# A radix search whose counts take several token groups per product: radices 64 and 32 in place of 41

## The chip, the cores and the metric

One NeuronCore of a Trainium2 chip. The metric is the device time of one execution in microseconds, the median of the runs; lower is better.

## The reference

Three stages follow one another. First a linear attention with decay over 4 x 8 heads, 768 positions and 48 dimensions per head. Its output, 3072 tokens of 384 features, goes to the second stage, a mixture of 8 experts with a greedy assignment: the (token, expert) logits are taken from the largest down, and each expert takes 384 tokens at most.

```python
logits = x @ w_gate
order = np.argsort(-logits.flatten())
for idx in order:
    tok, e = (int(idx) // E, int(idx) % E)
    if assigned[tok] >= 0 or counts[e] >= cap:
        continue
    assigned[tok] = e
    counts[e] += 1
...
    h = np.maximum(x[mask] @ w1[e], 0.0)
    out[mask] = h @ w2[e]
```

The third stage is a dense layer pair with hidden size 2048, `np.maximum(x @ w_in, 0)` squared, times `w_out`.

## The kernel before

The attention runs first, in 24 units of 128 tokens (4 sequences x 6 chunks). While it runs, the third stage's weights are loaded and split into a high and a low part, so that each later product is made of three (L1194, `three`: high x high, high x low, low x high). The logits of all 3072 tokens stay in SBUF as 128 partitions x 24 units x 8 experts.

**The routing** is done in rounds, `round_steps(q)` (L720). Each round finds the next expert that fills up. Every open token has its best open expert; the round looks for the largest key (the logit's 32 bits as an ordered integer, in two halves of 16 bits) at which some expert would hold 384 tokens. The search for one 16-bit half has three steps k = 0, 1, 2 with radix T = 41 and step sizes 1681, 41 and 1. The two halves give six search steps, called 0.0 to 1.2 here. One step is this:

- `compare(half, k)` (L783) on VectorE: thresholds (`steps` at k = 0, else `steps` plus the base found so far, L795), then 0/1 for "key at least threshold" in two operations of 12 units x 41 thresholds each (L802), written to `hot`, a bf16 tile of 24 x 128 columns per partition, of which a unit uses its first 41.
- `count(q, half, k)` (L1138) on TensorE: for each of the 24 units a product of the unit's 128 columns of `hot` with its 8 columns of `openc` (which expert an open token chose), summed in PSUM (L1143), and one product of `ones` with `need8` (L1144), which brings in the tokens already held and the capacity. Row t of the result says for each expert whether it would be full at threshold t.
- `fullness` (L805) on VectorE: 1 for each threshold at which some expert is full (`gecnt`, L808, with an accumulator read).
- `add_full` (L1146) on TensorE: a product that counts these thresholds on every partition (L1149).
- `rebase` (L810) on VectorE: the new base (L814, L817).

Step 1.0 has three more operations ahead of its comparison (L788 to L792). After step 1.2 come the sum per expert, the ranks of its tokens, and a permutation of 384 token numbers, with which GpSimd gathers the rows of x.

**Order of the work.** Round 0 runs alone between the attention and the first expert, each step waiting for the one before. Then `pe.Fori(0, E - 2)` runs `expert(i, False, True)` for six experts, each together with the search for the next one; the seventh expert has a round without search, the eighth none. In `expert` (L1258) the hidden groups g = 1 to 24 come in turn, 8 of the expert's first layer and 16 of the dense one. `hidden(i, g)` (L1200) is nine products of 384 columns (3 values of d, three each); `contract(i, g)` is nine more, into the outputs. The searching parts are written between them by hand: `count` of step g - 2 stands at the end of iteration g for g = 2 to 7, `add_full` of step g - 3 inside `hidden` for g = 3 to 8, as `between`, ahead of the three products of the last d (L1206). Group 8 is the first of the dense layer, and its products of each d wait for `x2_lo_ready`. VectorE's order is in `expert` from L969 on: `low(i, g)`, the low part of hidden group g, comes ahead of the search part of the same iteration; in iteration 7 the comparison of step 1.2 comes ahead of the three low parts of the dense layer's input (L986), and the fullness test of step 1.2 behind them.

```python
for k in range(3):
    last = pool.iota(steps[:, k, :], [[STEPS[k], T]], base=0, channel_multiplier=0, **iota)
...
pool.memset(hot[:, :, :], 0.0)
```

GpSimd makes these tables at the start (L369 to L376); VectorE and TensorE wait for `made` to reach 13, which the last of the three iotas does.

Of the kernel before, what the change touches and what calls it, by code (L numbers as in the profile page):

```python
# [27 lines left out]
E = 8  # L28
# [20 lines left out]
T = 41  # L49
STEPS = [T * T, T, 1]  # L50
# [14 lines left out]
def _route_names():  # L65

    names = ["best", "is_best", "ranked", "first", "choice", "open_choice", "held", "need",
             "sign", "key", "hi_int", "hi", "lo_int", "lo"]
    for half in range(2):
        if half:  # L70
            names += ["above", "clamp", "low_key"]
        for k in range(3):
            names += [f"thr{half}{k}"] if k else []
            names += [f"ge{half}{k}a", f"ge{half}{k}b", f"full{half}{k}", f"base{half}{k}"]
# [14 lines left out]
def build(nc, tt_d, nn_d, w_d, u_d, wg_d, we_d, m2_d, out_d):  # L89
# [5 lines left out]
    with ctx:  # L95
# [17 lines left out]
        full = sb("full", [P, 1], bf16)  # L113
        ones48 = sb("ones48", [P, 2 * NU], f32)
        steps = sb("steps", [P, 3, T], f32)
# [9 lines left out]
        ge = hot[:, :, 0:T]  # L125
# [58 lines left out]
        thr = sb("thr", [P, T], f32)  # L184
        gecnt = sb("gecnt", [T, E], f32)
# [25 lines left out]
        cnt_ps, n_ps, e_ps = rt_ps[:, 0:E], rt_ps[:, 16:17], rt_ps[:, 32:32 + E]  # L211
# [128 lines left out]
        def _(pool):  # L340
# [34 lines left out]
            pool.memset(hot[:, :, :], 0.0)  # L375
# [220 lines left out]
        def _(dve):  # L596
# [123 lines left out]
            def round_steps(q):  # L720
# [62 lines left out]
                def compare(half, k):  # L783

                    key = key2 if half else key_hi
                    if half and k == 0:

                        did("above", dve.tensor_scalar(tmp[:, :], key_hi[:, :], base[0][:, 0:1], 65536.0, ALU.subtract, ALU.mult))  # L788
                        after("above")
                        did("clamp", dve.tensor_scalar(tmp2[:, :], tmp[:, :], 65536.0, -65536.0, ALU.min, ALU.max))  # L790
                        after("clamp")
                        did("low_key", dve.tensor_tensor(key2[:, :], tmp2[:, :], key_lo[:, :], ALU.add))  # L792
                        after("low_key")
                    if k:
                        did(f"thr{half}{k}", dve.tensor_scalar(thr[:, :], steps[:, k, :], base[half][:, 0:1], None, ALU.add))  # L795
                        after(f"thr{half}{k}")
                        at = thr[:, :]
                    else:
                        at = steps[:, 0, :]
                    for part, units_ in (("a", slice(0, NU // 2)), ("b", slice(NU // 2, NU))):  # L800
                        did(f"ge{half}{k}{part}",
                            dve.tensor_tensor(ge[:, units_, :], key[:, units_].unsqueeze(2).broadcast_to([P, NU // 2, T]),  # L802
                                              at.unsqueeze(1).broadcast_to([P, NU // 2, T]), ALU.is_ge))

                def fullness(half, k):  # L805

                    dve.wait_ge(counted, 6 * q + 3 * half + k + 1)
                    did(f"full{half}{k}", dve.tensor_scalar(gecnt[:, :], cnt_ps[0:T, :], 0.0, None, ALU.is_ge, ALU.max, accum_out=full[0:T, :]))  # L808

                def rebase(half, k):  # L810

                    dve.wait_ge(summed, 6 * q + 3 * half + k + 1)
                    if k:
                        did(f"base{half}{k}", dve.tensor_scalar(base[half][:, :], n_ps, float(STEPS[k]), base[half][:, 0:1],  # L814
                                                                ALU.mult, ALU.add))
                    else:
                        did(f"base{half}{k}", dve.tensor_scalar(base[half][:, :], n_ps, float(STEPS[k]), None, ALU.mult))  # L817
# [214 lines left out]
        def _(pe):  # L1032
# [105 lines left out]
            def count(q, half, k):  # L1138

                for a in range(NU):  # L1140
                    if a % (NU // 2) == 0:
                        pe.wait_ge(route_done, q * RN + DONE[f"ge{half}{k}{'ab'[a // (NU // 2)]}"])
                    pe.matmul(cnt_ps, hot[:, a, :], openc[:, a, :], start=a == 0, stop=False)  # L1143
                pe.matmul(cnt_ps, ones[:, :], need8[:, :], start=False, stop=True).then_inc(counted, 1)  # L1144

            def add_full(q, half, k):  # L1146

                pe.wait_ge(route_done, q * RN + DONE[f"full{half}{k}"])
                pe.matmul(n_ps, ones_but0[:, :], full[:, :], start=True, stop=True).then_inc(summed, 1)  # L1149
# [44 lines left out]
            def three(out, hi_w, lo_w, hi_x, lo_x, first, last):  # L1194
# [141 lines left out]
```

## Time and profile before

| what | value |
|---|---|
| median of 3 runs | 878.4 us (878.37 to 878.81) |
| the profiled execution | 878.33 us, its span 876.6 us |
| TensorE busy | 811.8 us, 93% of the span |
| VectorE busy | 551.1 us, 63% |
| ScalarE and GpSimd busy | 290.0 and 328.7 us |
| attention | about 0 to 171 us |
| round 0 and the first gather | about 171 to 213 us |
| passes over the experts | from 213 us, some 82 us each |

The span is the time from the first to the last instruction of the profiled execution. Busy time of TensorE counts overlapping products once; single products last longer than the distance from one start to the next, so costs are read from distances between starts. The row of a group of the same instructions in the timeline gives their number as x24.

### The profile page before, as it was taken

The page shows a single profiled execution, that of the slowest core. Times are in us where ns is not written, and L with a number is a line of the kernel's source. Part 1 is how long each engine was busy: PE and PEld are TensorE (multiplying, and loading weights), DVE is VectorE, ACT ScalarE, POOL GpSimd, SP SyncE. Part 2 cuts the span into 40 slices and gives each one's busy share as a digit, 9 for nine tenths or more (in the row PEclk, how much of TensorE's full clock was granted, in tenths as well). Part 3 has the DMA queues.
Part 4 walks back from the last instruction along what each step waited for, and adds up shares of the span by engine and source line. Part 5 has one row for each costly group of instructions (what it writes and reads, how often), then busy time and mean ns, then how long its engine had stood idle before and what let it go on. Part 6 is the DMA issues. An engine that isn't in the chain of part 4 may idle for free.

```text
span 876.6 us, 18438 instructions
## 1 busy us (share of the span) xinstructions
PE 811.8 (93%) x6695; PEld 777.4 (89%) x6695; DVE 551.1 (63%) x1159; ACT 290.0 (33%) x581; POOL 328.7 (37%) x312
## 2 busy tenths in 40 slices
PE   5999999624999999999999999999999999999995
PEld 4888888623899999999999999999999999999995
DVE  7999999675777458546845692678358633931210
ACT  1233332103135315422542253235314533542332
POOL 6777677203026303520541063126303520531232
PEclk9999999855999999999999999999999999999998
DMA  8776776013023001200310040022002200400000
GB/s 228 213 220 232 214 250 209 29 51 121 2 73 100 26 2 72 99 27 0 120 50 27 8 162 0 27 72 99 9 18 72 99 27 1 172 1 28 1 1 27
DMA packets 22143, 69.86 MB, mean 80 GB/s; under 512 B 3552, under 2 KB 6752, under 8 KB 22112
## 3 DMA queue, kind: packets, MB, share of 16 engines
q1 hardware_dynamic: 19040, 59.99, 21.2%
q0 software_dynamic: 3072, 9.44, 3.1%
q8 instruction: 21, 0.34, 0.2%
q14 instruction: 10, 0.08, 0.0%
HBM read 59.98 MB, written 9.44 MB: 79 GB/s over the span
## 4 chain that ended last, share of the span: by engine, by line
PE 77%; DVE 11%; issue 5%; POOL 5%; ACT 1%; DMA 0%; DVEq 0%; POOLq 0%
PE bank L1196 16%; PE bank L1197 15%; PE bank L1198 15%; PE bank L1250 8%; PE bank L1252 8%; PE bank L1251 8%; PE bank L1143 3%; DVE ks L638 2%; PE bank L1059 2%; DVE am L645 1%; DVE rs L639 1%; POOL rku L401 1%; DVE hot L802 1%; POOL kn L385 1%; POOL rk L396 1%
## 5 line engine op out<-in xcount | busy, mean ns | idle before, releaser
L469 POOL TENSOR_TENSOR h_lo<-sq,h_hi 128x384 fp32r<-128x384 f32 x128 | 152.9, 1198 | 398.2 <-DVE sq L966 398.1
L966 DVE SCALAR_TENSOR_TENSOR sq<-bank,relu 128x384 f32<-128x384 f32 x128 | 71.0, 555 | 133.6 <-ACT relu L565 133.3
L1250 PE MATMUL bank<-m_hi,h_hi 128*128 128x384 f32 x384 | 132.0, 344 | 0.0
L1196 PE MATMUL bank<-x_hi,m_hi 128*128 128x384 f32 x384 | 130.6, 340 | 0.3
L1252 PE MATMUL bank<-m_hi,h_lo 128*128 128x384 f32 x384 | 129.8, 338 | 0.0
L1251 PE MATMUL bank<-m_lo,h_hi 128*128 128x384 f32 x384 | 129.5, 337 | 0.0
L1197 PE MATMUL bank<-x_lo,m_hi 128*128 128x384 f32 x384 | 129.2, 336 | 0.0
L1198 PE MATMUL bank<-x_hi,m_lo 128*128 128x384 f32 x384 | 129.1, 336 | 0.0
L565 ACT ACTIVATE relu<-bank 128x384 f32<-128x384 f32 x128 | 63.0, 492 | 194.5 <-PE bank L1198 192.3
L559 ACT ACTIVATE h_hi<-bank 128x384 fp32r<-128x384 f32 x64 | 31.5, 492 | 192.1 <-PE bank L1198 192.0
L958 DVE SCALAR_TENSOR_TENSOR h_lo<-bank,h_hi 128x384 fp32r<-128x384 f32 x64 | 35.4, 554 | 72.0 <-ACT h_hi L559 72.0
L1196 PEld LDWEIGHTS bank<-x_hi,m_hi 128*128 128x128 f32 x384 | 72.3, 188 | 1.1 <-DVE x_lo L986 0.9
L264 DVE TENSOR_TENSOR w_lo<-w_raw,w_hi 128x1024 fp32r<-128x1024 f32 x47 | 72.4, 1545 | 0.4 <-ACT w_hi L541 0.4
L1251 PEld LDWEIGHTS bank<-m_lo,h_hi 128*128 128x128 f32 x384 | 72.3, 188 | 0.0
L1250 PEld LDWEIGHTS bank<-m_hi,h_hi 128*128 128x128 f32 x384 | 72.2, 188 | 0.0
L1197 PEld LDWEIGHTS bank<-x_lo,m_hi 128*128 128x128 f32 x384 | 72.2, 188 | 0.0
L1252 PEld LDWEIGHTS bank<-m_hi,h_lo 128*128 128x128 f32 x384 | 72.2, 188 | 0.0
L1198 PEld LDWEIGHTS bank<-x_hi,m_lo 128*128 128x128 f32 x384 | 72.1, 188 | 0.0
L1196 PE MATMUL bank<-x_hi,w_hi 128*128 128x384 f32 x192 | 71.1, 370 | 0.8 <-DVE x_lo L923 0.8
L567 ACT ACTIVATE h_hi<-relu 128x384 fp32r<-128x384 f32 x128 | 67.4, 527 | 4.1
L1197 PE MATMUL bank<-x_lo,w_hi 128*128 128x384 f32 x192 | 65.7, 342 | 0.0
L1198 PE MATMUL bank<-x_hi,w_lo 128*128 128x384 f32 x192 | 65.7, 342 | 0.0
(172 smaller groups left out, 1572.4 us busy)
## 6 DMA issues: line engine op xcount, KB each, us to landing
w_raw<-we_in SPq DMA_DIRECT2D x48, 512.0 KB, 4.9
nn<-nn_in SPq DMA_DIRECT2D x24, 576.0 KB, 4.1
tt<-tt_in SPq DMA_DIRECT2D x48, 192.0 KB, 4.9
m_raw<-m_in SPq DMA_DIRECT2D x12, 512.0 KB, 5.7
x_rows<-yrow SPq DMA_DIRECT2D x24, 192.0 KB, 1.9
xg<-x_rows,perm_next POOLq DMA_INDIRECT x24, 4.4
out<-xg,perm_now POOLq DMA_INDIRECT x24, 2.6
u_row<-u_in SPq DMA_DIRECT2D x1, 192.0 KB, 6.0
```

The source lines that it names most:

```text
L264: eng.tensor_tensor(w_lo[:, cols], w_raw[j % W_SLOTS][:, :], w_hi[:, cols].bitcast(f32), ALU.subtract).then_inc(w_lo_ready, 1)
L469: pool.tensor_tensor(h_lo[g % 3][:, :], sq[g % 2][:, :], h_hi[g % 3][:, :].bitcast(f32), ALU.subtract).then_inc(lo2_ready, 1)
L565: act.activation(relu[:, :], h_ps[g % 3][:, 0:CAP], ACT.Relu).then_inc(relu_ready, 1)
L567: act.activation(h_hi[g % 3][:, :], relu[:, :], ACT.Square).then_inc(h_hi_ready, 1)
L958: dve.scalar_tensor_tensor(out=h_lo[g % 3][:, :], in0=h_ps[g % 3][:, 0:CAP], scalar=0.0, in1=h_hi[g % 3][:, :].bitcast(f32), op0=ALU.max, ...
L966: dve.scalar_tensor_tensor(out=sq[g % 2][:, :], in0=h_ps[g % 3][:, 0:CAP], scalar=0.0, in1=relu[:, :], op0=ALU.max, op1=ALU.mult).then_inc ...
L1196: pe.matmul(out, hi_w, hi_x, start=first, stop=False)
L1197: pe.matmul(out, hi_w, lo_x, start=False, stop=False)
L1198: return pe.matmul(out, lo_w, hi_x, start=False, stop=last)
L1250: pe.matmul(acc_ps[t][:, 0:DM], h_hi[r][:, s], m2_hi[:, c:c + DM], start=first, stop=False)
L1251: pe.matmul(acc_ps[t][:, 0:DM], h_hi[r][:, s], m2_lo[:, c:c + DM], start=False, stop=False)
L1252: last = pe.matmul(acc_ps[t][:, 0:DM], h_lo[r][:, s], m2_hi[:, c:c + DM], start=False, stop=end)
```

## The change

The radix is no longer the same in all steps. Steps 0.0 and 1.2 have radix 64, the other four radix 32; per half 64 x 32 x 32 = 65536 thresholds. The comparison writes its results to `hot` without gaps, t columns per unit. So 128 adjacent columns hold 2 units (radix 64) or 4 (radix 32), and one product takes these with the 16 or 32 columns of `openc` of the same units. Of its result only the diagonal blocks are wanted: rows j*t to (j+1)*t with columns 8j to 8j+8. A count has 12 or 6 such products and, as before, one with `need8`, into the first 8 columns. `fullness` first copies block 0 from PSUM to `folded`, then adds the others one by one, each operation waiting for the one before, and then makes the test on `folded`. The thresholds come from one `ramp` by multiplication, at k = 0 too. `full` gets a second column, for radix 64. The memset of `hot` goes. In `three` the call of `between` stands behind the first of the three products of the last d, one product later than before.

```diff
-T = 41
-STEPS = [T * T, T, 1]
+T = [[64, 32, 32], [32, 32, 64]]
+STEPS = [[1024, 32, 1], [2048, 64, 1]]
...
-            for k in range(3):
-                last = pool.iota(steps[:, k, :], [[STEPS[k], T]], base=0, channel_multiplier=0, **iota)
-            last.then_inc(made, 1)
+            pool.iota(ramp[:, :], [[1, 64]], base=0, channel_multiplier=0, **iota).then_inc(made, 1)
...
-            pool.memset(hot[:, :, :], 0.0)
...
+                    t = T[half][k]
                     if k:
-                        did(f"thr{half}{k}", dve.tensor_scalar(thr[:, :], steps[:, k, :], base[half][:, 0:1], None, ALU.add))
-                        after(f"thr{half}{k}")
-                        at = thr[:, :]
+                        did(f"thr{half}{k}", dve.tensor_scalar(thr[:, 0:t], ramp[:, 0:t], float(STEPS[half][k]), base[half][:, 0:1],
+                                                               ALU.mult, ALU.add))
                     else:
-                        at = steps[:, 0, :]
+                        did(f"thr{half}{k}", dve.tensor_scalar(thr[:, 0:t], ramp[:, 0:t], float(STEPS[half][k]), None, ALU.mult))
+                    after(f"thr{half}{k}")
+                    ge = flat[:, 0:NU * t].rearrange("p (u t) -> p u t", t=t)
...
                 def fullness(half, k):
+                    t = T[half][k]
                     dve.wait_ge(counted, 6 * q + 3 * half + k + 1)
-                    did(f"full{half}{k}", dve.tensor_scalar(gecnt[:, :], cnt_ps[0:T, :], 0.0, None, ALU.is_ge, ALU.max, accum_out=full[0:T, :]))
+                    did(f"fold{half}{k}0", dve.tensor_copy(folded[0:t, :], cnt_ps[0:t, 0:E]))
+                    for j in range(1, P // t):
+                        after(f"fold{half}{k}{j - 1}")
+                        did(f"fold{half}{k}{j}", dve.tensor_tensor(folded[0:t, :], cnt_ps[j * t:(j + 1) * t, j * E:(j + 1) * E],
+                                                                   folded[0:t, :], ALU.add))
+                    after(f"fold{half}{k}{P // t - 1}")
+                    did(f"full{half}{k}", dve.tensor_scalar(gecnt[0:t, :], folded[0:t, :], 0.0, None, ALU.is_ge, ALU.max,
+                                                            accum_out=full[0:t, t // 64:t // 64 + 1]))
...
             def count(q, half, k):
-                for a in range(NU):
+                many = P // T[half][k]
+                for a in range(0, NU, many):
                     if a % (NU // 2) == 0:
                         pe.wait_ge(route_done, q * RN + DONE[f"ge{half}{k}{'ab'[a // (NU // 2)]}"])
-                    pe.matmul(cnt_ps, hot[:, a, :], openc[:, a, :], start=a == 0, stop=False)
-                pe.matmul(cnt_ps, ones[:, :], need8[:, :], start=False, stop=True).then_inc(counted, 1)
+                    pe.matmul(cnt_ps[:, 0:many * E], flat[:, a * T[half][k]:a * T[half][k] + P],
+                              openc[:, a:a + many, :].rearrange("p u e -> p (u e)"), start=a == 0, stop=False)
+                pe.matmul(cnt_ps[:, 0:E], ones[:, :], need8[:, :], start=False, stop=True).then_inc(counted, 1)
...
                 pe.matmul(out, hi_w, hi_x, start=first, stop=False)
+                if between:
+                    between()
                 pe.matmul(out, hi_w, lo_x, start=False, stop=False)
...
-                    if between and d == DC - 1:
-                        between()
...
                     last = three(h_ps[h][:, 0:CAP], w1[:, c:c + P], w2[:, c:c + P], a1[:, d, :], a2[:, d, :],
-                                 d == 0, d == DC - 1)
+                                 d == 0, d == DC - 1, between if d == DC - 1 else None)
```

## Rows read from the trace of the kernel before

**Rows 1.** Second pass: stretch, us, PE, PEld, DVE, ACT, POOL busy, PEclk, DMA share, GB/s.
```profile
295.00:377.00 82.00, 82.00 (x624) 79.46 (x623) 52.52 (x124) 30.12 (x55) 26.39 (x23) 1.00 0.15 53
```

**Rows 2.** Timeline of TensorE, second pass, step 0.0: start us, us, engine, line, operation.
```profile
307.94 0.76 PE L1143 MATMUL bank<-openc,hot 128*128 128x8 bf16 x24
...
308.56 0.17 PE L1144 MATMUL bank<-need,ones 128*128 128x8 bf16 x1
...
309.56 0.34 PE L1198 MATMUL bank<-x_hi,w_lo 128*128 128x384 f32 x1
...
309.74 0.18 PE L1149 MATMUL bank<-full,ones_but 128*128 128x1 bf16 x1
```

**Rows 3.** Timeline of TensorE, second pass, the ranks' products.
```profile
338.54 0.20 PE L1158 MATMUL bank<-cand,before 128*128 128x48 bf16 x1
...
338.60 0.43 PE L1250 MATMUL bank<-m_hi,h_hi 128*128 128x384 f32 x1
```

**Rows 4.** Groups of VectorE by form: busy us, mean ns | idle before.
```profile
L802 DVE TENSOR_TENSOR hot<-key_hi,thr 128x492 bf16<-128x492 f32 x28 | 17.6, 673 | 0.5
...
L745 DVE TENSOR_TENSOR r<-logits,best 128x192 f32<-128x192 f32 x8 | 2.9, 358 | 0.3
```

**Rows 5.** Timeline of VectorE, second pass, steps 0.0 and 0.1.
```profile
306.27 1.25 DVE L802 TENSOR_TENSOR hot<-key_hi,steps 128x492 bf16<-128x492 f32 x2
...
308.76 0.16 DVE L808 TENSOR_SCALAR_CACHE_REDUCE gecnt<-bank 41x8 f32<-41x8 f32 x1 [0.77 <-PE bank L1144]
...
310.43 1.26 DVE L802 TENSOR_TENSOR hot<-key_hi,thr 128x492 bf16<-128x492 f32 x2
```

**Rows 6.** Timeline of TensorE and VectorE, second pass, step 1.0.
```profile
317.80 0.18 PE L1149 MATMUL bank<-full,ones_but 128*128 128x1 bf16 x1
...
318.02 0.22 DVE L814 TENSOR_SCALAR base<-bank,base 128x1 f32<-128x1 f32 x1 [1.02 <-PE bank L1149]
...
318.27 0.24 DVE L788 TENSOR_SCALAR tmp<-key_hi,base 128x24 f32<-128x24 f32 x1
...
318.98 1.26 DVE L802 TENSOR_TENSOR hot<-key,steps 128x492 bf16<-128x492 f32 x2
...
320.04 0.76 PE L1143 MATMUL bank<-openc,hot 128*128 128x8 bf16 x24
```

**Rows 7.** Timeline of VectorE ahead of the loop, small operations behind the last step.
```profile
191.07 0.17 DVE L831 SCALAR_TENSOR_TENSOR row<-bank,rank 128x8 f32<-128x8 f32 x1 [0.31 <-PE bank L1154]
...
191.27 0.16 DVE L834 TENSOR_REDUCE top<-row 128x1 f32<-128x8 f32 x1
```

**Rows 8.** Timeline of both engines, first pass, step 0.0.
```profile
224.33 1.25 DVE L802 TENSOR_TENSOR hot<-key_hi,steps 128x492 bf16<-128x492 f32 x2
...
225.63 0.37 PEld L1143 LDWEIGHTS bank<-openc,hot 128*128 128x128 bf16 x12 [0.21 <-DVE hot L802]
...
225.92 0.10 PEld L1144 LDWEIGHTS bank<-need,ones 128*128 128x128 bf16 x1
```

**Rows 9.** Timeline ahead of the loop, step 0.1: test and add_full.
```profile
177.14 0.16 DVE L808 TENSOR_SCALAR_CACHE_REDUCE gecnt<-bank 41x8 f32<-41x8 f32 x1 [0.60 <-PE bank L1144]
...
177.37 0.19 PE L1149 MATMUL bank<-full,ones_but 128*128 128x1 bf16 x1 [0.26 <-DVE gecnt L808]
```

**Rows 10.** Timeline of both engines, second pass, step 1.2.
```profile
327.98 1.26 DVE L802 TENSOR_TENSOR hot<-key,thr 128x492 bf16<-128x492 f32 x2
...
329.34 1.60 DVE L986 TENSOR_TENSOR x_lo<-bank,x_hi 128x384 fp32r<-128x384 f32 x3
...
329.67 0.76 PE L1143 MATMUL bank<-openc,hot 128*128 128x8 bf16 x24
...
331.45 0.18 PE L1149 MATMUL bank<-full,ones_but 128*128 128x1 bf16 x1
```

**Rows 11.** Timeline of the start, GpSimd and VectorE.
```profile
6.34 0.43 POOL L370 IOTA steps<- 128x41 f32 x3
...
6.89 1.61 DVE L622 TENSOR_TENSOR_SCAN powr<-w_s,powr,zeros 112x128 f32<-112x128 f32 x4 [1.35 <-POOL steps L370]
```

More of the change, by code:

```diff
@@ L72, in _route_names @@
         for k in range(3):
-            names += [f"thr{half}{k}"] if k else []
-            names += [f"ge{half}{k}a", f"ge{half}{k}b", f"full{half}{k}", f"base{half}{k}"]
+            names += [f"thr{half}{k}", f"ge{half}{k}a", f"ge{half}{k}b"]
+            names += [f"fold{half}{k}{j}" for j in range(P // T[half][k])]
+            names += [f"full{half}{k}", f"base{half}{k}"]
     names += ["at_least", "reached", "reached_sum",
@@ L112, in build @@
         ones_but0 = sb("ones_but0", [P, P], bf16)
-        full = sb("full", [P, 1], bf16)
+        full = sb("full", [P, 2], bf16)
         ones48 = sb("ones48", [P, 2 * NU], f32)
-        steps = sb("steps", [P, 3, T], f32)
+        ramp = sb("ramp", [P, 64], f32)
         rank8 = sb("rank8", [P, E], f32)
@@ L124, in build @@
         hot = sb("hot", [P, NU, P], bf16)
-        ge = hot[:, :, 0:T]
+        flat = hot[:, :, :].rearrange("p u s -> p (u s)")
         att = ExitStack()
@@ L183, in build @@
         need8 = sb("need8", [P, E], bf16)
-        thr = sb("thr", [P, T], f32)
-        gecnt = sb("gecnt", [T, E], f32)
+        thr = sb("thr", [P, 64], f32)
+        gecnt = sb("gecnt", [64, E], f32)
+        folded = sb("folded", [64, E], f32)
         base = [sb(f"base{j}", [P, 1], f32) for j in range(2)]
@@ L813, in rebase @@
                     if k:
-                        did(f"base{half}{k}", dve.tensor_scalar(base[half][:, :], n_ps, float(STEPS[k]), base[half][:, 0:1],
+                        did(f"base{half}{k}", dve.tensor_scalar(base[half][:, :], n_ps, float(STEPS[half][k]), base[half][:, 0:1],
                                                                 ALU.mult, ALU.add))
                     else:
-                        did(f"base{half}{k}", dve.tensor_scalar(base[half][:, :], n_ps, float(STEPS[k]), None, ALU.mult))
+                        did(f"base{half}{k}", dve.tensor_scalar(base[half][:, :], n_ps, float(STEPS[half][k]), None, ALU.mult))
                     after(f"base{half}{k}")
@@ L1138, in count @@
             def count(q, half, k):
-                for a in range(NU):
+                many = P // T[half][k]
+                for a in range(0, NU, many):
                     if a % (NU // 2) == 0:
                         pe.wait_ge(route_done, q * RN + DONE[f"ge{half}{k}{'ab'[a // (NU // 2)]}"])
-                    pe.matmul(cnt_ps, hot[:, a, :], openc[:, a, :], start=a == 0, stop=False)
-                pe.matmul(cnt_ps, ones[:, :], need8[:, :], start=False, stop=True).then_inc(counted, 1)
+                    pe.matmul(cnt_ps[:, 0:many * E], flat[:, a * T[half][k]:a * T[half][k] + P],
+                              openc[:, a:a + many, :].rearrange("p u e -> p (u e)"), start=a == 0, stop=False)
+                pe.matmul(cnt_ps[:, 0:E], ones[:, :], need8[:, :], start=False, stop=True).then_inc(counted, 1)
             def add_full(q, half, k):
                 pe.wait_ge(route_done, q * RN + DONE[f"full{half}{k}"])
-                pe.matmul(n_ps, ones_but0[:, :], full[:, :], start=True, stop=True).then_inc(summed, 1)
+                wide = T[half][k] // 64
+                pe.matmul(n_ps, ones_but0[:, :], full[:, wide:wide + 1], start=True, stop=True).then_inc(summed, 1)
             def expert_counts(q):
@@ L1192, in _, with three @@
                         last.then_inc(x_sum, 1)
-            def three(out, hi_w, lo_w, hi_x, lo_x, first, last):
+            def three(out, hi_w, lo_w, hi_x, lo_x, first, last, between=None):
                 pe.matmul(out, hi_w, hi_x, start=first, stop=False)
+                if between:
+                    between()
                 pe.matmul(out, hi_w, lo_x, start=False, stop=False)
```

6 lines of the change are left out of this document (3 added, 3 removed).

## The prediction

> **What bounds the kernel now.** I read the busy time by stretches first. In a full pass over one expert TensorE is busy for 82.00 of 82.00 us [rows 1], with VectorE at 52.5: there an instruction taken off TensorE is time taken off the end, as long as VectorE keeps up. Then I read the timeline of TensorE around one search step of the second pass [rows 2]. A search step is a count, VectorE's fullness test, add_full, the rebase and the next comparison; I call the six 0.0 to 1.2 (half, k). The 24 count products take 0.62 us from the first start to the start of the product with ones, 26 ns each, and add_full starts 1.18 us after the latter. Neighbouring 384-column products start 0.18 us apart. So a count costs TensorE far less than the 0.17 us that one product lasts. Last I read VectorE's side, for where it is late next: step 0.0, step 1.0, step 1.2, the first pass, and the serial search ahead of the loop.
>
> **What goes from TensorE.** Counts with radix 32 issue 6 products in place of 24, those with radix 64 issue 12. If a product of 16 or 32 columns is as dear as one of 8, a pass saves 4 x 18 + 2 x 12 = 96 products of 26 ns, 2.48 us, and six searching passes 14.9 us. Two products with 48 columns in the same stretch take 0.06 us together until the next product starts [rows 3], 30 ns each; narrower ones should lie between 26 and 30, and I take 26. At 30 the 48 that are left cost 0.2 us more a pass.
>
> **What VectorE gets.** Per comparison the elements go from 2 x 492 to 2 x 384 or 2 x 768. An operation on 192 elements lasts 358 ns and one on 492 lasts 673 [rows 4], 1.05 ns per element more; the two halves of 492 last 1.25 us together [rows 5], so the second starts 0.09 before the first one's end. That gives 0.56 us for one half with radix 32 and 1.03 for the pair, and 0.96 and 1.83 with radix 64. Steps 0.0 and 1.0 get a threshold operation that they did not have; three chained small operations ahead of step 1.0's comparison take 318.98 - 318.27 = 0.71 us [rows 6], so 0.24.
>
> The fullness test gets a fold in front: four chained operations with radix 32, two with radix 64, and the trace has none that read the counts from partitions 32, 64 or 96. From below, the nearest row is an 8-element operation that reads the PSUM bank: the one that depends on it starts 0.20 us later [rows 7]. From above, the rebase with its pointer operand gives 0.25 [rows 6]. I take 0.20, since the folds have the shape of the former and no pointer, and keep 0.25 for the range; below, nothing in the chain could be shorter than some 0.15, the 0.17 that such an operation lasts less its overlap.
>
> The Trainium skill (VectorE: DVE Perf Modes, Rules for kernel authors) speaks against a change of this sort: the count of chained VectorE operations is what matters, not their semaphores. The table in its section on the errata gives 120 cycles and the elements for a PSUM source, 133 ns here by estimate; the rows show 0.20. With its figure the search ahead of the loop would be 1.3 us shorter than below and step 1.2 some 0.13 in each pass, and the time about 872.0.
>
> **The search ahead of the loop** is serial, so each operation counts in full. After a comparison ends, the second half of the products starts 0.05 us later [rows 8] and takes 0.31, half of the 0.62 above; add_full starts 0.23 after the test [rows 9]. With radix 32: comparison -0.22, the second half of the products 12 to 3, -0.23, folds +0.80, together +0.35. With radix 64: +0.58, -0.16, +0.40, together +0.82. Four and two of them and two thresholds: 1.40 + 1.64 + 0.48 = **3.5 us lost**. The gather and the expert's load hang on its result and move with it.
>
> **The loop**, step by step.
> Steps 0.1, 0.2 and 1.1: the test starts 0.20 us after the product with ones (308.76 less 308.56) [rows 2, 5], so with the folds add_full can start 0.20 + 0.80 + 0.23 = 1.23 after it. TensorE came there after 1.18; now one 384-column product more is issued ahead of it (the call moves into three(), behind its first product), so 1.36, and the chain is hidden with 0.13 to spare. That product covers it: without it TensorE would wait 0.05. The next comparison starts 0.69 after add_full (310.43 less 309.74, and 0.06 more behind a pointer rebase) [rows 2, 5] and is done with 1.03 + 0.05 at about 1.83, ahead of the count's second half at some 2.1. So these three keep 0.46 each, 1.39.
> Step 1.0: before, the product with ones starts 2.86 us after add_full (317.80 to 320.04 and 0.62) [rows 6]; with the moved add_full and the shorter count it could be 2.86 - 0.18 - 0.46 = 2.22. But the comparison starts 1.18 after add_full, now 1.42, and 1.03 + 0.05 and three products later it is 2.58. TensorE waits 0.36 and 0.10 is left. Queued behind the comparison is the low part of hidden group 5, which is due an entire group later.
> Step 0.0: the comparison starts at 306.27 [rows 5], now at 306.51; it ends at 308.34, and the six products of the second half bring the product with ones to 308.55, against 308.56 before. The saving of 0.31 is eaten whole.
> Step 1.2: the comparison starts at 327.98 and holds VectorE until 329.72 instead of 329.24 [rows 10]. Behind it in VectorE's order are the three low parts of the second layer's input, for which TensorE waits at hidden group 8. The first now starts at 329.72 in place of 329.34, and group 8 starts about 0.3 later than it could. The three take 0.47 each and are through at 331.13, two folds bring the test to 331.53 and add_full to 331.76, against 331.45. One product less follows it, so this step **loses 0.14**. The sum over experts comes only behind the nine products of group 9 and is not held up.
> A pass so gains 0 + 1.39 + 0.10 - 0.14 = 1.35 us, six of them 8.1. In the first pass VectorE is late already: step 0.0's comparison starts at 224.33 and TensorE, waiting, reaches the product with ones at 225.92 [rows 8]. Now that is 224.33 + 0.24 + 1.83 + 0.05 + 0.16 = 226.61, another 0.69 lost. The loop gains **7.4 us**.
>
> **The start.** GpSimd makes one ramp, not three step tables: two of three iotas that take 0.43 us together go, and VectorE waits on the last of them [rows 11]. 0.28 us gained. The memset of the one-hot tile that goes lies behind that, under VectorE's own work: nothing; were it on the path it would be a gain. The pass without search and the last one have no counts.
>
> **Sum.** -0.28 + 3.5 - 7.4 = -4.2 us. The profiled execution took 878.33 us, 1.7 around its span of 876.6; it stands 0.07 under the median of the runs. I forecast **874.1 us**.
>
> **Rivals.**
> *The fold is dearer than I take it, and the kernel slower.* With a fold step of 0.20 + x, the twenty folds ahead of the loop cost 20x; in a pass the four steps with radix 32 stall by 4x - 0.13 each and step 1.2 by 2x, so six passes cost 108x - 3.1. The gain is gone at 128x - 3.1 = 4.2, x = 0.057: it decides at a step of 0.257 us. At 0.30, which reads from other partitions than it writes could cause, the time is 878.3 - 4.2 + 9.7 = 883.8. For it: no row shows such an operation, and TensorE's spare is 0.13 us. Against it: the small operations of the rows lie between 0.20 and 0.25 apart. 8 in 100.
> *No change that can be told.* A fold step of 0.25 gives 128 x 0.05 - 3.1 = +3.3, 877.4 us; products at 30 ns and waits that cost TensorE 0.1 more at each of three stalls lead there too. 13 in 100.
> *The waits that I find at steps 0.0, 1.0 and 1.2 do not cost time.* Then the whole 14.9 less 3.5 is kept with the start, 866.7 us. It would need VectorE to do 768 elements in the time of 492, for which no row speaks. 5 in 100.
> That the products are not fewer can be excluded: the loop's stride sets their number.
>
> **How the numbers follow.** My own case has 74 in 100, all of it faster by more than 0.2% (1.8 us, about what a measurement of this kernel can tell from no change). With the third rival that is 0.79 faster, 0.13 the same, 0.08 slower. The range runs from 870.7, where a fold step is 0.15 (1.0 less ahead of the loop, 0.6 less in it, from step 1.2 alone) and the waits at steps 0.0 and 1.2 halve (1.8 less), to 877.4 at a fold step of 0.25; it leaves out the first rival, the third and a sliver.
>
> **What would show it.** TensorE's counts: 12 or 6 products to a count, still 26 ns apart; in radix-32 steps 0.16 us from the first to the product with ones. VectorE: comparisons of 384 elements near 0.56 us and of 768 near 0.96; folds starting 0.20 apart. Waits of TensorE: new ones on the comparison at steps 0.0 and 1.0 of every pass (0.3 to 0.4 us), at group 8 on the low part of its input (0.3), and none at add_full in steps 0.1, 0.2 and 1.1. The search ahead of the loop from the first comparison to the last rebase longer by 3.5 us, each searching pass shorter by 1.35. A wait at add_full in every step, or folds over 0.25 apart, would make me wrong.

## The result and the profile after

The changed kernel takes 873.11 us (median of 5 runs, 873.04 to 875.22) against 878.4 (878.29 to 878.81): a ratio of 0.9948, interval 0.9936 to 0.996, so 0.5% faster. The profiled execution took 873.07 us with a span of 871.3; before it was 878.33 with 876.6. The runs of the changed kernel and of some variants fall on two levels some 2 us apart, so small differences are read from the profiled executions, which but for six_idle_ops lie on the lower level, and not from the medians.

From the page of the changed kernel: busy time and chain.

```profile
span 871.3 us, 17377 instructions
...
PE 798.1 (92%) x6023; PEld 761.6 (87%) x6023; DVE 575.3 (66%) x1313; ACT 290.8 (33%) x581; POOL 328.8 (38%) x309
...
q14 instruction: 11, 0.09, 0.0%
...
PE 69%; DVE 15%; issue 8%; POOL 5%; ACT 1%; DMA 0%; DVEq 0%; POOLq 0%; ACTq 0%
```

TensorE has 672 products fewer and 13.7 us less busy time, VectorE 154 operations and 24.2 us more. TensorE gave up far more than the 5.3 us by which the kernel is faster; the rest is idle time of TensorE, 2.9 us of it because the search ahead of the loop takes longer. The stretch that answers to [rows 1], with the same columns:

```profile
295.00:377.00 82.00, 81.55 (x536) 78.71 (x535) 56.46 (x147) 31.25 (x57) 26.94 (x24) 1.00 0.15 53
```

TensorE is no longer busy for all of it: 0.45 us of idle time is new. Where it lies, the timeline of TensorE in the second pass shows, beside [rows 2, 6, 10].

```profile
310.32 0.74 PE L1153 MATMUL bank<-openc,hot 128*128 128x16 bf16 x12
310.92 0.17 PE L1155 MATMUL bank<-need,ones 128*128 128x8 bf16 x1
...
312.26 0.18 PE L1161 MATMUL bank<-full,ones_but 128*128 128x1 bf16 x1
...
314.30 0.32 PE L1153 MATMUL bank<-openc,hot 128*128 128x32 bf16 x6
314.47 0.17 PE L1155 MATMUL bank<-need,ones 128*128 128x8 bf16 x1
...
315.81 0.18 PE L1161 MATMUL bank<-full,ones_but 128*128 128x1 bf16 x1
...
321.39 0.24 PE L1153 MATMUL bank<-openc,hot 128*128 128x32 bf16 x3
321.82 0.24 PE L1153 MATMUL bank<-openc,hot 128*128 128x32 bf16 x3 [0.19 <-DVE hot L803]
321.91 0.17 PE L1155 MATMUL bank<-need,ones 128*128 128x8 bf16 x1
...
330.42 0.54 PE L1153 MATMUL bank<-openc,hot 128*128 128x16 bf16 x12
330.81 0.17 PE L1155 MATMUL bank<-need,ones 128*128 128x8 bf16 x1
...
332.51 0.18 PE L1161 MATMUL bank<-full,ones_but 128*128 128x1 bf16 x1
```

With radix 32 a count takes 0.17 us (314.30 to 314.47) where 24 products took 0.62 [rows 2]: still 26 to 28 ns a product, at 32 columns as at 8. At step 0.0 the count is cut in two by the comparison and lasts 0.60, as long as before; at step 1.0 the halves start 0.43 apart, where three products take 0.08. The weight loads show the third wait, in step 1.2:

```profile
331.12 0.19 PEld L1208 LDWEIGHTS bank<-x_hi,m_hi 128*128 128x128 f32 x1 [0.23 <-DVE x_lo L995]
...
332.51 0.10 PEld L1161 LDWEIGHTS bank<-full,ones_but 128*128 128x128 bf16 x1 [0.22 <-DVE gecnt L816]
```

The other side is VectorE's timeline of the same pass, beside [rows 5].

```profile
308.65 0.19 DVE L798 TENSOR_SCALAR thr<-ramp 128x64 f32<-128x64 f32 x1
308.87 1.82 DVE L803 TENSOR_TENSOR hot<-key_hi,thr 128x768 bf16<-128x768 f32 x2
...
314.67 0.15 DVE L810 COPY folded<-bank 32x8 f32<-32x8 f32 x1 [0.23 <-PE bank L1155]
314.86 0.55 DVE L813 TENSOR_TENSOR folded<-bank,folded 32x8 f32<-32x8 f32 x3
315.45 0.15 DVE L816 TENSOR_SCALAR_CACHE_REDUCE gecnt<-folded 32x8 f32<-32x8 f32 x1
...
320.53 0.18 DVE L798 TENSOR_SCALAR thr<-ramp 128x32 f32<-128x32 f32 x1
320.74 1.03 DVE L803 TENSOR_TENSOR hot<-key,thr 128x384 bf16<-128x384 f32 x2
...
328.77 1.83 DVE L803 TENSOR_TENSOR hot<-key,thr 128x768 bf16<-128x768 f32 x2
330.51 1.48 DVE L995 TENSOR_TENSOR x_lo<-bank,x_hi 128x384 fp32r<-128x384 f32 x3
```

The comparisons last 1.03 and 1.83 us a pair, the four folds 0.78 (314.67 to 315.45), 0.19 each. Ahead of the loop nothing lies beside the folds (both engines, step 0.1 of round 0, beside [rows 9]):

```profile
177.22 0.17 PE L1155 MATMUL bank<-need,ones 128*128 128x8 bf16 x1
177.43 0.15 DVE L810 COPY folded<-bank 32x8 f32<-32x8 f32 x1 [0.37 <-PE bank L1155]
...
178.42 0.19 PE L1161 MATMUL bank<-full,ones_but 128*128 128x1 bf16 x1 [1.03 <-DVE gecnt L816]
```

Distances from one product with ones to the next, then from that of step 1.2 to the next pass's (us), and the period:

| kernel | 0.0-0.1 | 0.1-0.2 | 0.2-1.0 | 1.0-1.1 | 1.1-1.2 | 1.2-0.0 | pass |
|---|---|---|---|---|---|---|---|
| before | 4.03 | 4.03 | 4.04 | 4.03 | 5.59 | 60.92 | 82.64 |
| after | 3.55 | 3.54 | 3.90 | 3.56 | 5.34 | 61.23 | 81.13 |

(The pass is the mean of the five periods from the first pass's product of step 0.0 to the sixth's, the other columns are of the second pass. Step 0.1 in the text is the column 0.0-0.1, and so on.)

### The profile page after: what moved, and what is told of

It reads as the page before. It is cut to its first block, busy times and chain, and to the rows that moved or that the text cites. A ratio compares the mean times of both kernels' runs of the same rounds, so it can differ in the third digit from the quotient of the medians.

```text
span 871.3 us, 17377 instructions
## 1 busy us (share of the span) xinstructions
PE 798.1 (92%) x6023; PEld 761.6 (87%) x6023; DVE 575.3 (66%) x1313; ACT 290.8 (33%) x581; POOL 328.8 (38%) x309
## 4 chain that ended last, share of the span: by engine, by line
PE 69%; DVE 15%; issue 8%; POOL 5%; ACT 1%; DMA 0%; DVEq 0%; POOLq 0%; ACTq 0%
PE bank L1208 14%; PE bank L1211 13%; PE bank L1212 13%; PE bank L1262 8%; PE bank L1264 8%; PE bank L1263 8%; DVE hot L803 2%; DVE ks L637 2%; PE bank L1068 2%; DVE am L644 1%; DVE rs L638 1%; POOL rku L400 1%; POOL kn L384 1%; PE bank L1153 1%; POOL rk L395 1%
## 5 line engine op out<-in xcount | busy, mean ns | idle before, releaser
L1208 PE MATMUL bank<-x_hi,w_hi 128*128 128x384 f32 x192 | 68.4, 356 | 0.8 <-DVE x_lo L932 0.8
L1211 PE MATMUL bank<-x_lo,w_hi 128*128 128x384 f32 x192 | 68.2, 355 | 0.0
```

## The experiments

All were timed against the kernel before, on the same chip: 878.53 us for the first four, 878.49 for the second four, 878.41 for the last. Diffs are against the changed kernel unless the text says otherwise. Loop start is the first expert product.

| kernel | us | ratio, interval | span | loop start | first ones 0.0 | pass |
|---|---|---|---|---|---|---|
| before | 878.4 | | 876.6 | 212.99 | 225.95 | 82.64 |
| after | 873.11 | 0.9948, 0.9936 to 0.996 | 871.3 | 215.93 | 229.78 | 81.13 |
| products_24 | 885.59 | 1.0083, 1.0067 to 1.01 | 884.0 | 217.83 | 231.77 | 82.93 |
| move_undone | 875.9 | 0.9965, 0.9951 to 0.9979 | 872.5 | 215.97 | 229.83 | 81.32 |
| move_alone | 878.67 | 1.0002, 0.9992 to 1.0011 | 877.2 | 213.44 | 226.38 | 82.66 |
| one_fold_more | 894.03 | 1.0177, 1.016 to 1.0194 | 891.4 | 217.48 | 231.05 | 84.46 |
| six_idle_ops | 898.64 | 1.0227, 1.0213 to 1.0241 | 896.9 | 217.04 | 230.65 | 85.52 |
| swap_half0 | 873.48 | 0.9942, 0.9929 to 0.9956 | 871.7 | 215.97 | 228.93 | 81.26 |
| first_tables | 874.91 | 0.9962, 0.9948 to 0.9975 | 873.1 | 215.59 | 229.07 | 81.32 |
| tables_keys | 874.3 | 0.9953, 0.9939 to 0.9966 | 872.4 | 215.47 | 228.95 | 81.22 |
| tables_keys_tree | 875.55 | 0.9965, 0.9952 to 0.9979 | 874.3 | 216.63 | 230.09 | 81.33 |
| pad_384 | 879.5 | 1.0006, 0.9997 to 1.0015 | 876.5 | 216.28 | 230.15 | 81.74 |
| one_ramp | 870.04 | 0.9905, 0.989 to 0.992 | 868.3 | 215.66 | 229.14 | 80.70 |
| one_ramp_keys | 869.9 | 0.9904, 0.9889 to 0.9919 | 867.7 | 215.41 | 228.74 | 80.64 |

**products_24: the fewer products given back.**

```diff
+                    for _ in range(many - 1):
+                        pe.matmul(spare_ps[:, 0:many * E], flat[...], openc[...], start=True, stop=True)
```

> The changed kernel in which each count product is issued 2 or 4 times, the repeats into unused columns of another bank, so that TensorE has 24 products per count again; radices, folds and all else stay. My account: 26 ns each where TensorE is the one that is late: 0.46 in steps 0.1, 0.2 and 1.1, 0.23 in 1.0 (second half), 0.16 in 0.0, nothing in 1.2, where TensorE waits for VectorE anyway; 1.8 a pass, 11 in six, 1.3 ahead of the loop: 885 us, slower than the kernel before. Rival: the gain is not from the number of products but from something else of the change (thresholds, comparison's dense layout, the place of add_full): 873 to 876.

As my theory had it: 885.59. With 24 products again and everything else as in the changed kernel, the first four steps take 4.01, 4.01, 4.16 and 4.01 us. Three of them are as long as before the change within 0.02 us; step 1.0 is 0.12 longer, which it is in move_alone below too, so that is the price of the later add_full. So the whole gain of the change is the products that go, and without it the new VectorE work makes the kernel 0.8% slower than before. Of the 1.9 us by which the loop starts later than in the changed kernel, 1.3 are the search, as expected; 0.5 lie ahead of it, where nothing was changed: the attention ends a few tenths of a us earlier or later from one kernel to the next.

**move_undone and move_alone: the place of add_full.** The call of `between` put back, and moved in the kernel before.

```diff
-                if between:
-                    between()
...
+                    if between and d == DC - 1:
+                        between()
```

> The changed kernel with add_full back ahead of the last d. My account: the fold chain is ready 1.20 us after the product with ones and TensorE arrives after 1.17, so each radix-32 step waits 0.03; step 1.0's comparison starts 0.13 earlier and its wait shrinks by that; at step 1.2 add_full is bound by the folds behind the low parts, and one product more follows it, +0.17. Together +0.16 a pass, 874 us. Rival: the later place is what hides the fold, and without it TensorE waits 0.2 or more at add_full in all six steps: 880 us or more.

> The kernel before with only the later place of add_full. My account: the chain from add_full to the next comparison starts 0.17 later; only step 1.0 has no slack for it (0.06), so TensorE waits 0.1 there in each of six passes: 879.1 us against 878.4, a difference hardly to be told. Rival: the place alone brings part of the gain (add_full used to cost TensorE a gap): 876 or less.

By the profiled executions the move is worth 0.2 us a pass, 1.2 in all; the median of move_undone stands 2.8 above the changed kernel's, but its runs reach from 874.11 to 876.28, and the lowest ones of the two stand 1.1 apart. Its rows from TensorE's timeline, steps 0.0 and 0.1:

```profile
311.14 0.17 PE L1155 MATMUL bank<-need,ones 128*128 128x8 bf16 x1
312.32 0.18 PE L1161 MATMUL bank<-full,ones_but 128*128 128x1 bf16 x1
314.72 0.17 PE L1155 MATMUL bank<-need,ones 128*128 128x8 bf16 x1
315.92 0.18 PE L1161 MATMUL bank<-full,ones_but 128*128 128x1 bf16 x1
```

In step 0.1 add_full now starts 1.20 after the product with ones in place of 1.18: the folds are just late, the steps 0.1, 0.2 and 1.1 take 3.58 to 3.61 in place of 3.54 to 3.56, and at step 1.2 one more product is left behind add_full. Step 1.0 alone gets shorter, 3.76 in place of 3.90, since its comparison hangs on add_full. In the kernel before, where add_full never waits for the test, the move gives nothing in all: step 1.0 gets 0.12 longer (4.16), the others 0.02 shorter, and the pass takes 82.66 in place of 82.64.

**one_fold_more: one dependent operation more per step.**

```diff
-                    did(f"full{half}{k}", dve.tensor_scalar(gecnt[0:t, :], folded[0:t, :], ...
+                    did(f"more{half}{k}", dve.tensor_copy(folded2[0:t, :], folded[0:t, :]))
+                    after(f"more{half}{k}")
+                    did(f"full{half}{k}", dve.tensor_scalar(gecnt[0:t, :], folded2[0:t, :], ...
```

> The changed kernel with one more chained operation of 8 elements (a copy of the folded counts) ahead of the fullness test in every step. My account: 0.19 each; six of them in full ahead of the loop, +1.1; in a pass the spare of 0.15 at steps 0.1, 0.2 and 1.1 takes most of it (0.04 each), some 0.1 at step 1.0, nothing at 0.0 and 0.19 at 1.2, +0.4 a pass; together +3.6, 876.7 us. Rival A: the folds are wholly hidden in the loop: +1.1, 874.2. Rival B: they are on TensorE's path in each step: +1.1 + 36 x 0.19 = +8, 881.

A miss, by 17 us. The steps did what was expected: in the radix-32 steps add_full comes 1.39 to 1.42 behind the product with ones in place of 1.34 to 1.36, and round 0 is longer by 1.2 us (1.1 expected). The loss is elsewhere. The waits of VectorE, longest sums (us in total, times, longest), have one that the changed kernel has not:

```profile
DVE best L743 <- issue: 12.6, 5, 2.7
```

From the second pass on VectorE stands still for about 2.5 us ahead of the first operation of each pass, waiting for nothing that the profile shows, and the instruction queue has moved 0.29 MB in 36 packets in place of 0.09 in 11:

```profile
q14 instruction: 36, 0.29, 0.1%
```

The third pass shows what that costs: both engines' timelines, and then the stretch behind it (columns as in rows 1).

```profile
393.19 0.35 DVE L743 TENSOR_REDUCE best<-logits 128x24 f32<-128x192 f32 x1 [2.45 <-issue]
```

```profile
398.77 0.31 PE L1156 MATMUL bank<-openc,hot 128*128 128x16 bf16 x6 [0.91 <-DVE hot L804]
399.64 0.31 PE L1156 MATMUL bank<-openc,hot 128*128 128x16 bf16 x6 [0.56 <-DVE hot L804]
```

```profile
402.00:404.90 2.90, 2.90 (x16) 2.60 (x15) 1.33 (x3) 0.49 (x1) 0.00 (x0) 0.52 0.00 0
```

The comparison of step 0.0 comes late, TensorE waits 1.5 us for it, and then the granted clock falls to 0.52, nearly the 1.2 GHz level, for some 3 us: step 0.0 to 0.1 takes 5.11 us in place of 3.55, in four of the six passes. By the timeline of TensorE the 20 us are 11 for the five stops, 6 for the four stretches of low clock, and most of the rest the folds. Two causes of the stops were possible: six operations more in the body of VectorE's loop, or six more in the search.

**six_idle_ops: as many operations more, off the search.** Six copies, each waiting for the one before, behind the comparisons with the slot numbers.

```diff
+                    for j in range(6):
+                        after(f"idle{j - 1}" if j else "slot_hot2")
+                        did(f"idle{j}", dve.tensor_copy(folded2[:, :], folded[:, :]))
```

> The changed kernel with six small copies more on VectorE in every round, each waiting for the one before, as many as one_fold_more has and with its tile, but behind the comparisons with the slot numbers, where no product waits for them at once. Theory (one_fold_more lost its time because six instructions more made VectorE's loop body too long, so that its instructions are fetched again in each pass): VectorE stands still for about 2.5 us at the first operation of the later passes again, with three times as many packets on the instruction queue, and the time is 888 or more. Rival (the loss came from where the six copies stood in the search): no such stop, and 873 to 875.

The stops do not depend on where the six stand. The steps behind step 0.0 are as in the changed kernel (3.55, 3.91, 3.56, 5.34), and yet it takes 898.64 us, with the same wait and again 36 packets and 0.29 MB on the instruction queue:

```profile
DVE best L744 <- issue: 12.5, 5, 2.8
```

The tile that both variants add is not the cause: tables_keys_tree below has it too, with two operations a round more than the changed kernel in place of six, and it has no such wait, 11 packets and 0.09 MB. The start times of the queue's packets in the traces say what is moved: the changed kernel fetches packets of 8 KB up to 305.5 us, just after VectorE has begun the second pass of the loop, and then none until 710 us, behind the loop; in one_fold_more and six_idle_ops five come in each of the third to sixth passes, one of them during each stop. So instructions are fetched again in every pass, and between two and six operations more than the changed kernel has lies an edge.

The expectation was wrong in one point: something does wait for the six copies. TensorE waits 1.2 us in each pass for GpSimd, whose work VectorE's copies push back (first pass), a wait that neither the changed kernel nor one_fold_more has.

```profile
281.78 0.44 PE L1267 MATMUL bank<-m_hi,h_hi 128*128 128x384 f32 x1 [1.22 <-POOL h_lo L470]
```

Seven such waits cost 8 us, three stretches of low clock behind step 0.0 some 5 (5.1 us in place of 3.55, in the first, fourth and fifth pass), and the five stops about 11, as in one_fold_more.

**swap_half0: radix 64 at step 0.1 in place of 0.0.**

```diff
-T = [[64, 32, 32], [32, 32, 64]]
-STEPS = [[1024, 32, 1], [2048, 64, 1]]
+T = [[32, 64, 32], [32, 32, 64]]
+STEPS = [[2048, 32, 1], [2048, 64, 1]]
```

> The changed kernel with radix 64 in step 0.1 in place of 0.0 (32, 64, 32). My account: step 0.0 is then bound by TensorE and 0.44 shorter; step 0.1's comparison of 2 x 768 elements makes TensorE wait, +0.51; together +0.07 a pass; in the first pass, where VectorE is late at step 0.0, 0.87 less and 0.51 more. Sum about 0: 873.1 us, with the wait moved from step 0.0 to 0.1. Rival: the wait at step 0.0 is not set by the comparison's length, and it stays while step 0.1 gets a new one: 875.5.

As expected, 873.48: the stretch up to step 0.0 gets 0.44 us shorter and the step to 0.1 0.54 longer (4.09), where TensorE now waits 0.24 for the longer comparison. The wait goes where the 768 elements go.

**first_tables, tables_keys, tables_keys_tree: VectorE relieved.** Two tables of first thresholds made at the start, so that steps 0.0 and 1.0 need no threshold operation; then also the low half of the key behind the comparison of step 0.0; then also the four blocks added as a tree.

```diff
+        first_steps = [sb(f"first_steps{j}", [P, T[j][0]], f32) for j in range(2)]
...
-                        did(f"thr{half}{k}", dve.tensor_scalar(thr[:, 0:t], ramp[:, 0:t], float(STEPS[half][k]), None, ALU.mult))
+                        at = first_steps[half][:, :]
```

> The changed kernel with the thresholds of steps 0.0 and 1.0 as two tables that GpSimd makes at the start, behind the semaphore that others wait for, so that VectorE issues no threshold operation there. My account: the comparison of steps 0.0 and 1.0 starts 0.22 earlier and TensorE's wait there shrinks by as much; 0.44 a pass, 2.6 in six, 0.44 ahead of the loop: 870.1 us. Rival: something else ends the wait at these steps (ScalarE's high part, a DMA): 872.6, only what is saved ahead of the loop.

> As first_tables, and the two operations that make the low half of the key stand behind the comparison of step 0.0, which doesn't need them. My account: that comparison starts 0.17 earlier still; of its wait of 0.29 the tables take 0.22, so 0.07 a pass is left to gain, 0.17 in the first pass, where VectorE is later, and 0.2 ahead of the loop, where the two operations now lie in VectorE's wait for the count: 869.4 us. Rival: they push the low part of hidden group 2 and the fold back, and nothing is gained: 870.1.

> As tables_keys, and the four-block fold as a tree: two copies that don't depend on each other, two adds, one last add, five operations in place of four but a shorter chain (0.66 in place of 0.77 us if independent ones start 0.09 apart). My account: 0.1 in each of four steps ahead of the loop, nothing in the loop, where the chain is hidden: 869.0 us. Rival: it is the number of operations that counts, not their dependence, and it is 0.1 longer per step: 869.9.

Three misses of 5 to 7 us. In first_tables the waits shrank as they should: loop start 0.34 earlier, first product with ones 0.71, step 1.0 3.70 in place of 3.90. But the 384-column products behind them came slower: from add_full of step 1.2 to the next pass 59.89 us, where the changed kernel takes 59.53. The tree is worse than the chain: its step takes 5 operations, 0.95 us from the first to the test in place of 0.78. The second copy in it depends on nothing and still starts 0.19 us behind the first (step 0.1 ahead of the loop):

```profile
177.55 0.15 DVE L824 COPY folded<-bank 32x8 f32<-32x8 f32 x1 [0.37 <-PE bank L1179]
177.74 0.16 DVE L832 COPY folded<-bank 32x8 f32<-32x8 f32 x1
```

So among these reads of the counts it is the number of operations that counts. It is not so for every small operation. Three others of the changed kernel, with no wait between them, start 0.10 us apart:

```profile
271.24 0.18 DVE L917 TENSOR_TENSOR tmp<-tmp,gt 128x24 f32<-128x24 f32 x1
271.34 0.17 DVE L918 SCALAR_TENSOR_TENSOR closed<-fill,closed 128x8 f32<-128x8 f32 x1
271.44 0.16 DVE L920 TENSOR_SCALAR row<-fill 128x8 f32<-128x8 f32 x1
```

They read no PSUM, and the tree's copies read it from different partitions; which of the two makes the difference was not tried.

**pad_384: an unused tile.** The two tables had moved every tile behind them by 384 bytes. This kernel has the tile and no instruction changed.

```diff
         ramp = sb("ramp", [P, 64], f32)
+        pad = sb("pad", [P, 96], f32)
```

> The changed kernel with one unused tile of 384 bytes a partition where first_tables has its two tables, and not one instruction more or less. Theory (the place of the tiles sets the pace of the products): the products of the passes run slower by 0.4 to 0.5 us a pass, in all eight: 876.5. Rival (the place of the tiles has no part in it): 873.1, with the same 59.53 us from the last threshold count of a pass to the next ones product.

The pad alone costs 5.2 us by the span, about the whole gain of the change (6.4 by the median; the lowest runs of the two stand 4.9 apart). It is more than the theory had: 0.6 us a pass in place of 0.4 to 0.5, and 0.35 us ahead of them, no more than the attention's end differs between kernels anyway. The page's groups of products, changed kernel first, then pad_384 (busy us, mean ns):

```profile
L1262 PE MATMUL bank<-m_hi,h_hi 128*128 128x384 f32 x384 | 131.9, 343 | 0.0
L1208 PE MATMUL bank<-x_hi,m_hi 128*128 128x384 f32 x384 | 130.0, 339 | 1.1
...
L1211 PE MATMUL bank<-x_lo,m_hi 128*128 128x384 f32 x384 | 129.5, 337 | 0.0
...
L1212 PE MATMUL bank<-x_hi,m_lo 128*128 128x384 f32 x384 | 128.9, 336 | 0.0
```

```profile
L1263 PE MATMUL bank<-m_hi,h_hi 128*128 128x384 f32 x384 | 133.0, 346 | 0.0
...
L1209 PE MATMUL bank<-x_hi,m_hi 128*128 128x384 f32 x384 | 131.6, 343 | 1.1
L1212 PE MATMUL bank<-x_lo,m_hi 128*128 128x384 f32 x384 | 130.8, 341 | 0.0
...
L1213 PE MATMUL bank<-x_hi,m_lo 128*128 128x384 f32 x384 | 130.1, 339 | 0.0
```

These four forms are 1.1 to 1.6 us busier for the same 384 products; the two others of the dense layer (m_lo,h_hi and m_hi,h_lo) only 0.1 and 0.3. The six forms together have 779.3 us in the changed kernel, 784.9 with the pad. first_tables has 784.9 too, so its loss is the pad's. The change under study also moves tiles, but is not touched by this: the kernel before has 780.2, move_undone 779.5, move_alone 779.4.

**one_ramp and one_ramp_keys: the same relief without a tile.** The ramp holds multiples of 1024 and serves as the table of both first steps.

```diff
-            pool.iota(ramp[:, :], [[1, 64]], ...
+            pool.iota(ramp[:, :], [[RAMP, 64]], ...
...
-                        did(f"thr{half}{k}", dve.tensor_scalar(thr[:, 0:t], ramp[:, 0:t], float(STEPS[half][k]), None, ALU.mult))
+                        every = STEPS[half][k] // RAMP
+                        at = ramp[:, 0:t * every:every]
```

> The changed kernel with its ramp written in multiples of 1024, so that the ramp itself is the threshold table of steps 0.0 and 1.0 and their threshold operation falls away, as in first_tables, but with no tile and no iota more. Theory (in first_tables the waits shrank and the products behind them ran slower because an extra 384 byte tile had shifted every tile behind it): with the tiles where the changed kernel has them, the gain of about 0.22 us at each of steps 0.0 and 1.0 stays, 0.44 a pass and 2.6 in six, and 0.44 ahead of the loop: 870.3, with 59.5 us from the last threshold count of a pass to the ones product of the next. Rival (an earlier comparison itself makes the later products slower, wherever the tiles lie): 59.9 for that stretch and 874.8.

> one_ramp with the two operations on the low half of the key behind the comparison of step 0.0, as in tables_keys. By the theory of the shifted tiles 0.1 us less at step 0.0 of each pass and 0.3 to 0.6 ahead of the loop: 869.6, which would be the shortest of all. By the rival 874.3.

870.04 and 869.9 us, 1.0% faster than before and better than both kernels of the study. From add_full of step 1.2 to the next pass's product with ones it takes 59.3 us, less than the changed kernel's 59.53 since the comparison comes earlier, where first_tables took 59.89: the earlier comparison does not slow the products, the place of the tiles does. TensorE's timeline of one_ramp, second pass:

```profile
309.47 0.52 PE L1157 MATMUL bank<-openc,hot 128*128 128x16 bf16 x12
309.85 0.17 PE L1159 MATMUL bank<-need,ones 128*128 128x8 bf16 x1
...
320.33 0.47 PE L1157 MATMUL bank<-openc,hot 128*128 128x32 bf16 x6
320.65 0.17 PE L1159 MATMUL bank<-need,ones 128*128 128x8 bf16 x1
```

The count of step 0.0 takes 0.38 us in place of 0.60 and that of step 1.0 0.32 in place of 0.52. The low keys bring 0.06 us more a pass and 0.25 to 0.4 ahead of it; the medians of the two can't be told apart.

## Why the prediction was right

I forecast 874.1 us and faster; it was 873.11. By the profiled executions the last product ends 5.3 us earlier (861.36 against 866.66), where my sum had 4.2. Of the 1.1 us that the sum was short, 0.3 lie ahead of the loop and 1.0 in the passes, with 0.2 the other way in the first one. Two of the five runs took 875.1 and 875.2 us; that the median is 873.11 and not one of these is luck, though they lie in my range too.

- **Products by their distance.** Right: 26 to 28 ns from 8 to 32 columns, and products_24 returned the steps to their old length.
- **Comparisons and folds.** Right: 1.03 and 1.83 us a pair, as interpolated. The fold was taken at 0.20 between 0.15 and 0.25; it is 0.19. On the rule weighed there: the table of the Trainium skill (VectorE: DVE Perf Modes, the section on the errata) gives 133 ns by estimate for such an operation; the measured distance is 0.19 and decides. Its other statement, that the count of chained operations is what matters, the tree bears out for the folds: five operations with a shorter chain took 0.17 us more than four.
- **Search ahead of the loop.** Taken as 3.5; it is 3.2. From the first threshold operation to the last rebase 20.04 us (172.24 to 192.28) against 16.84; a radix-32 step got 0.29 longer in place of 0.35. The four folds at 0.78 in place of 0.80 and a test to add_full of 0.22 in place of 0.23 are about half of the difference.
- **The start.** 0.28 taken, 0.26 measured: the scan starts at 6.63 in place of 6.89, and the search as much earlier. But products_24 and pad_384, with the same start, begin their search 0.5 and 0.3 us later than the changed kernel, so this term can't be told from what moves the attention's end by itself.
- **Steps 0.1, 0.2, 1.1.** 0.46 each taken; 0.48, 0.49 and 0.47 measured. The moved product does cover the folds: its spare was given as 0.05 short without it, and move_undone shows add_full 0.02 late and the steps 0.03 to 0.06 longer.
- **Step 0.0.** Nothing kept was taken, 0.05 measured: 59.53 us from add_full of step 1.2 to the product with ones, against 59.75 before, of which 0.17 is the product that no longer follows add_full. The count takes 0.60 from its first product to that with ones, against 0.62.
- **Step 1.0.** 0.10 taken, 0.14 measured, and the wait lies where it was put, ahead of the second half of the count.
- **Step 1.2.** A loss of 0.14 taken, 0.11 measured, with the wait at group 8 (0.23 against 0.3 expected) and add_full 1.70 behind the product with ones. (Its working sets 329.72, an end less the overlap, beside 329.24, an end; the loss itself was worked out from the low part's start at 329.34 and does not change.)
- **A pass.** 1.35 taken, 1.51 measured. The difference, 1.0 us in six, is the largest error of the sum, of small terms that all fell to the same side.
- **First pass.** 0.69 taken, 0.89 measured (first product with ones 3.83 later, loop start 2.94): 0.2 more. A stop of VectorE by 0.29 us in the keys would account for it; it is there in this pass alone and in no pass of the kernel before. Why it stops there was not tried.

What the sum did not contain: operations more in VectorE's loop were priced only by their own time and by the waits they cause. one_fold_more shows that six more cost 20 us, 17 of them by another way, which no row of the kernel before shows. The change itself added 22 operations a round to the same loop and stayed below that edge; that it did is luck, since the prediction did not ask.

## What to carry to other kernels

Cost small products by the distance between their starts, not by their duration, and check which engine then ends each stretch: here 13.7 us less TensorE time bought 5.3. Before adding even idle instructions to a long loop body, and after adding a tile, compare the instruction queue and the mean duration of untouched products; both can cost more than the change that is being measured. When an improvement does not show in the time though its waits have gone, compare the pace of the instructions that nobody touched.

## What the runs showed of the hardware

- **A loop body can be too long for VectorE.** Six small operations more, in either of two places in the body, and VectorE stops for 2.4 to 2.8 us once in each of the five later passes, with 25 more packets and 0.20 MB more on the instruction queue. The stops cost TensorE about 11 us in each of the two variants, of 21 and 26 in all. With two operations more there is none of it. That a packet of this queue starts during each stop, and five in a pass where the changed kernel has none, says that instructions are fetched again. The Trainium skill (Advanced Engine Details and Errata, ISA Cache) has a rule of this kind: 32 KB, in two lines of 16 KB or 256 instructions each, outside TensorE. No run here shows the size or the line; that there is an edge, and that 96 products more a pass on TensorE (products_24) bring no such stop, agrees.
- **A short wait of TensorE can cost more than itself.** The 1.5 us wait at step 0.0 was followed by a granted clock of 0.52 over some 3 us, another 1.6 us lost, after four of the five stops of one_fold_more. In six_idle_ops, with the same wait (0.9 and 0.6 us) in all six passes, it fell in three, one of them the first, ahead of any stop of VectorE. Waits of 0.2 to 0.3 us in the changed kernel leave it at 1.00, and so did 1.2 and 0.6 us in its first pass, so the length of the wait is not all that decides.
- **The place of the tiles sets the pace of the products.** 384 bytes between tiles make the 384-column products of the dense layer 0.7% busier (784.9 us against 779.3), some forms 1.2%, others not. The small tile that one_fold_more adds lies behind the operands of these products, and their pace stayed. Which tile has to lie where was not tried, and the cause stays open.
